# Weight remainders of the first nine chunks on TensorE and ScalarE, x(0) loaded in three parts, the second network's splits in block 1

## The reference

```python
w = np.exp(weight_gen - max); w = w / (w.sum(-1) + 1e-9)      # 8 heads x 7 taps
out[b,s,h] = sum_k w[b,s,h,k] * x_pad[b, s+k, h]              # x_pad: 6 zero rows ahead
xn = out / np.sqrt(np.mean(out * out, -1) + 1e-6) * rms_g
y = (silu(xn @ w_gate) * (xn @ w_val)) @ w_out                # 192 -> 1536 -> 192
h = y @ w_in                                                  # 192 -> 2048
z = (h * sigmoid(1.702 * h)) @ w_out2                         # 2048 -> 192
```

## Time and profile before

| | us |
|---|---|
| median of 3 runs (lowest, highest) | 1263.56 (1263.46, 1265.49) |
| profiled execution | 1263.64 |
| its span | 1261.9 |
| PE busy in the span | 1216.1 (96%) |
| DVE, ACT, POOL busy | 788.4, 680.8, 68.5 |

### The profile page before, as it was taken

The page is one execution under the profiler, slowest core; times in us unless marked ns, Lnnn a source line. Parts: engine busy times, 40 slices in busy tenths (PEclk is TensorE's granted clock), DMA queues, the critical chain, the costliest instruction groups (busy, mean ns, idle before and its releaser), DMA issues.

```text
span 1261.9 us, 28865 instructions
## 1 busy us (share of the span) xinstructions
PE 1216.1 (96%) x11968; PEld 1063.5 (84%) x11968; DVE 788.4 (62%) x1218; ACT 680.8 (54%) x1222; POOL 68.5 (5%) x67
## 2 busy tenths in 40 slices
PE   0889999999999999999999999999999999999998
PEld 0769999999888898988889888898988889888888
DVE  8868566484855749476474856648476574854532
ACT  3364655546465554656556455554656555464554
POOL 3760000000000000000000000000000000000000
PEclk9989999999999999999999999999999999999999
DMA  6230000010100001001010100001000000000000
GB/s 191 79 94 32 1 18 33 18 33 1 33 18 18 32 5 45 2 17 34 18 33 1 49 1 18 32 17 34 1 18 32 18 32 2 14 2 14 1 14 14
DMA packets 14625, 33.69 MB, mean 27 GB/s; under 512 B 1828, under 2 KB 7842, under 8 KB 14496
## 3 DMA queue, kind: packets, MB, share of 16 engines
q1 hardware_dynamic: 14496, 31.85, 7.8%
HBM read 25.55 MB, written 6.29 MB: 25 GB/s over the span
## 4 chain that ended last, share of the span: by engine, by line
PE 93%; DVE 4%; issue 1%; ACT 1%; POOL 1%; DMA 0%; SPq 0%; DVEq 0%; POOLq 0%; ACTq 0%
PE up_ps L808 49%; PE acc L808 37%; PE acc L812 4%; PE up_ps L812 3%; DVE mixed L627 1%; DVE tap L623 1%; DVE hidden L758 1%; DMA x_win<-in_x_dram 0%; DVE h_lo L767 0%; DVE normed_all L623 0%; POOL pair_lo L413 0%; PE acc L1051 0%; POOL out_w L413 0%; DVE mixed L623 0%; ACT up_w L446 0%
## 5 line engine op out<-in xcount | busy, mean ns | idle before, releaser
L767 DVE TENSOR_TENSOR h_lo<-hidden,h_hi 128x512 fp32r<-128x512 f32 x448 | 312.3, 697 | 359.2 <-ACT h_hi L545 357.7
L545 ACT CAST h_hi<-hidden 128x512 fp32r<-128x512 f32 x448 | 278.1, 621 | 250.1 <-DVE hidden L758 240.5
L808 PE MATMUL acc<-out_w,h_hi 64*128 64x384 f32 x1024 | 302.6, 355 | 1.0 <-DVE out_sb L714 1.0
L812 PE MATMUL acc<-out_w,h_hi 64*128 64x384 f32 x1024 | 302.4, 355 | 0.0
L538 ACT ACTIVATE hidden<-up_ps 128x512 f32<-128x512 f32 x256 | 152.7, 596 | 194.4 <-PE up_ps L812 194.3
L808 PE MATMUL acc<-out_w,h_lo 64*128 64x192 f32 x1024 | 255.0, 249 | 0.0
L812 PE MATMUL acc<-out_w,h_lo 64*128 64x192 f32 x1024 | 254.7, 249 | 0.0
L812 PE MATMUL up_ps<-x_hi,up_w 64*128 64x512 f32 x752 | 237.0, 394 | 0.0
L808 PE MATMUL up_ps<-x_hi,up_w 64*128 64x512 f32 x752 | 236.8, 394 | 0.0
L808 PE MATMUL acc<-h_hi,out_w 64*128 64x512 f32 x576 | 196.8, 394 | 9.1 <-POOL pair_lo L413 6.5
L812 PE MATMUL acc<-h_hi,out_w 64*128 64x512 f32 x576 | 197.4, 396 | 0.1
(11 more groups left out here) (111 smaller groups left out, 3219.2 us busy)
## 6 DMA issues: line engine op xcount, KB each, us to landing
x_win<-in_x_dram SPq DMA_DIRECT2D x14, 960.0 KB
out_dram<-out_sb SPq DMA_DIRECT2D x15, 384.0 KB, 2.3
stage<-in_moe_w_out_dram SPq DMA_DIRECT2D x13, 192.0 KB, 2.5
logits<-in_weight_gen_dram SPq DMA_DIRECT2D x16, 112.0 KB, 2.0
stage<-in_moe_w_in_dram SPq DMA_DIRECT2D x4, 256.0 KB, 2.6
stage<-in_moe_w_in_dram SPq DMA_DIRECT2D x8, 128.0 KB, 3.1
stage<-in_moe_w_gate_dram SPq DMA_DIRECT2D x3, 256.0 KB, 2.8
stage<-in_moe_w_gate_dram SPq DMA_DIRECT2D x6, 128.0 KB, 3.2
```

What stands on the lines that cost most here:

```text
L545: nc.scalar.copy(h_hi[:, u % 4, :], hidden[:, u % 2, :]).then_inc(hi_ready, 1)
L767: nc.vector.tensor_tensor(h_lo[:, u % 4, :], hidden[:, u % 2, :], h_hi[:, u % 4, :].bitcast(F32), ALU.subtract).then_inc(lo_ready, 1)
L808: return nc.tensor.matmul(ps, w[TOP], data[TOP], start=start, stop=stop)
L812: return nc.tensor.matmul(ps, w[LOW], data[LOW], start=start, stop=stop)
```

## The change

1. Chunks 0 to 8 (`BY_PE`): the remainder is no longer GpSimd's. TensorE multiplies the staged fp32 chunk by the identity into a bank of `up_ps` and adds the rounded chunk times the negated identity (`leave`), and ScalarE copies the bank to the `lo` tile (`chunk_lo`). On ScalarE rounding n alternates with remainder n - 1. GpSimd makes the negated identity and splits chunks 9 to 17 once x(0) is scaled.
2. x(0) comes in three parts (own rows; the three rows next to them; the three farthest), and its taps are mixed in reverse order, so that a tap waits for no more than it reads. A rest chunk is one transfer.
3. The mean is gone from VectorE: GpSimd adds the epsilon to the sum of squares ahead of its power, and g is scaled by the root of 192 once.
4. The main part of x(0) is turned and scaled before the rest part; its twin copy moves from VectorE to ScalarE. The first two taps of x(1) stand ahead of unit 0; the squares (6 to 5) and the turn of x(1) (10 to 9) move up by a unit.
5. The second network's chunks (18 to 33) are split in block 1, behind GpSimd's power for x(2). The last eight are loaded and rounded there too, behind the loads of x(2) and x(3) on SP; the first eight are rounded one to a unit in block 0.

```diff
     for k in range(2, TAPS):
         MIX += [f"mul{k}", f"add{k - 1}"]
-    MIX += [f"add{TAPS - 1}", "mean", "scale"]
+    MIX += [f"add{TAPS - 1}", "scale"]
...
-        return 48 * (g + 1) if g < 2 else g * 16 + 80
+        return 32 if g == 0 else g * 16 + 64
...
-                5: ["mul4", "add3"], 6: ["mul5", "add4"], 7: ["mul6", "add5"], 8: ["add6"], 9: ["mean"],
-                10: ["scale"]}
-    MIX_SLOT_0 = {0: ["mul0", "mul1"], 1: ["mul2", "add1"], 2: ["mul3", "add2"], 3: ["mul4", "add3"],
-                  4: ["mul5", "add4"], 5: ["mul6", "add5"], 6: ["add6"], 7: ["mean"], 8: ["scale"]}
-    EVAC_O, EVAC_Y0, SQUARE_0, SQUARE, SPLIT_Y, X_T = 1, 1, 6, 8, 8, U1 - 1
+                5: ["mul4", "add3"], 6: ["mul5", "add4"], 7: ["mul6", "add5"], 8: ["add6"], 10: ["scale"]}
+    AHEAD = ["mul0", "mul1"]
+    MIX_SLOT_0 = {0: ["mul2", "add1"], 1: ["mul3", "add2"], 2: ["mul4", "add3"], 3: ["mul5", "add4"],
+                  4: ["mul6", "add5"], 5: ["add6"], 7: ["scale"]}
+    EVAC_O, EVAC_Y0, SQUARE_0, SQUARE, SPLIT_Y, X_T = 1, 1, 5, 8, 8, U1 - 1
...
+    BY_PE = 9
+    HELD = CHUNKS1 + SLOTS
+    TURN_1 = U1 - 3
...
+    def hi_before(u):
+        if u < 0:
+            return SLOTS + LENT
+        return min(SLOTS + LENT + 2 * u + 2, CHUNKS1 + max(u - 2, 1), HELD)
...
+        def left_bank(n):
+            return up_ps[(n + 3) % 4]
...
+            def load_first_x():
+                sp.dma_start(x_win[:, HALO:, :], x_v[:, 0:STEP, :]).then_inc(own_in, 16)
+                for first, end, loaded in ((HALO // 2, HALO, near_in), (0, HALO // 2, x_in)):
+                    for b in range(B):
+                        lo, hi = b * BATCH_P, (b + 1) * BATCH_P - 1
+                        sp.dma_start(x_win[lo + 1:hi + 1, first:end, :],
+                                     x_v[lo:hi, OWN - HALO + first:OWN - HALO + end, :]).then_inc(loaded, 16)
...
-                    for half in range(2):
-                        sp.dma_start(to[half * REST:(half + 1) * REST, :],
-                                     w[P:D, c * COLS:(c + 1) * COLS]).then_inc(loaded, 16)
+                    twice = w[P:D, c * COLS:(c + 1) * COLS].unsqueeze(0).broadcast_to([2, REST, COLS])
+                    sp.dma_start(to, twice).then_inc(loaded, 16)
...
-            load_first_x(1)
+            load_second_x()
             load_logits(2)
-            for n in range(SLOTS + LENT, CHUNKS1 + SLOTS):
+            for n in range(SLOTS + LENT, HELD):
                 load_chunk(n)
             load_x(2)
-            for n in range(CHUNKS1 + SLOTS, len(chunks)):
-                load_chunk(n)
             load_logits(3)
             load_x(3)
+            for n in range(HELD, len(chunks)):
+                load_chunk(n)
             for i in range(2, GROUPS - 2):
...
+            pool.wait_ge(ident_ready, 1)
+            nc.gpsimd.tensor_scalar_mul(neg_ident[:, :], ident[:, :], -1.0).then_inc(neg_ready, 1)
+            pool.wait_ge(g_in, 48)
+            nc.gpsimd.tensor_scalar_mul(g_main[:, :], g_main[:, :], math.sqrt(D)).then_inc(g_ready, 1)
+            nc.gpsimd.tensor_scalar_mul(g_rest[:, :], g_rest[:, :], math.sqrt(D)).then_inc(g_ready, 1)
...
+            def rms(g):
+                pool.wait_ge(squared, g * STEP + STEP)
+                if g:
+                    pool.wait_ge(mix, mix_count(g - 1, "scale"))
+                nc.gpsimd.tensor_scalar_add(rms_stat[:, 1, :], rms_stat[:, 0, :], D * 1e-6).then_inc(summed, 1)
+                pool.wait_ge(summed, g + 1)
+                nc.gpsimd.tensor_tensor(rms_stat[:, 2, :], rms_stat[:, 1, :], neg_half[:, :],
+                                        ALU.pow).then_inc(rstd, 1)
+            rms(0)
+            pool.wait_ge(mix, mix_count(0, "scale"))
+            for n in range(BY_PE, CHUNKS1):
                 split_chunk(n)
-            pool.wait_ge(chunk_split, RMS0_AT)
-            rms(0)
-            pool.wait_ge(rstd, 1)
-            for n in range(RMS0_AT, RMS1_AT):
+            rms(1)
+            rms(2)
+            for n in range(CHUNKS1, len(chunks)):
                 split_chunk(n)
-            pool.wait_ge(chunk_split, RMS1_AT)
-            rms(1)
-            pool.wait_ge(rstd, 2)
-            for n in range(RMS1_AT, len(chunks)):
-                split_chunk(n)
-            pool.wait_ge(chunk_split, len(chunks))
-            for g in range(2, GROUPS):
+            for g in range(3, GROUPS):
                 rms(g)
...
+            def chunk_lo(n):
+                _, kind, t, _ = chunks[n]
+                act.wait_ge(chunk_left, n + 1)
+                for _, _, lo, f, _ in split_parts(left_bank(n)[:, :], kind, t):
+                    last = nc.scalar.copy(lo, f)
+                last.then_inc(chunk_split, 1)
...
+                else:
+                    act.wait_ge(rest_scaled, 1)
+                    nc.scalar.copy(y_twin[REST:P, :], x_f32[0:REST, 1, :]).then_inc(twin_ready, 1)
...
-                        for n in range(SLOTS + LENT + 2 * u, min(SLOTS + LENT + 2 * u + 2, len(chunks))):
+                        for n in range(hi_before(u - 1), hi_before(u)):
                             chunk_hi_half(n)
+                    if i == 1 and U1 <= u < U1 + len(chunks) - HELD:
+                        chunk_hi_half(HELD + u - U1)
...
-            for n in range(SLOTS + LENT - 4):
+            chunk_hi_half(0)
+            for n in range(1, BY_PE - 2):
                 chunk_hi_half(n)
+                chunk_lo(n - 1)
             mix_square(0)
             mix_exp(1)
-            for n in range(SLOTS + LENT - 4, SLOTS + LENT):
-                chunk_hi_half(n)
-            act.wait_ge(g_in, 48)
+            chunk_lo(BY_PE - 3)
+            chunk_hi_half(BY_PE - 2)
+            chunk_hi_half(BY_PE - 1)
+            act.wait_ge(g_ready, 2)
             scale_main(0)
             round_first(0)
+            chunk_lo(BY_PE - 2)
+            chunk_lo(BY_PE - 1)
+            for n in range(BY_PE, SLOTS + LENT):
+                chunk_hi_half(n)
...
+                        dve.wait_ge(soft, soft_count(g, "norm"))
+                    if g == 0 and k == 0:
+                        dve.wait_ge(own_in, 16)
+                    if g == 0 and k == 1:
+                        dve.wait_ge(near_in, 16 * B)
+                    if k == (HALO // 2 + 1 if g == 0 else 0):
                         dve.wait_ge(x_in, x_count(g))
-                        dve.wait_ge(soft, soft_count(g, "norm"))
                     if k == 3 and g:
...
-                    ins = nc.vector.tensor_tensor(*tap_product(to, k, 0, STEP), ALU.mult)
+                    ins = nc.vector.tensor_tensor(*tap_product(to, k if g else TAPS - 1 - k, 0, STEP), ALU.mult)
...
-            for step in MIX[:-2]:
+            for step in MIX[:-1]:
                 mix_step(0, step)
             mix_step(1, "max")
             mix_step(1, "sub")
-            mix_step(0, "mean")
             mix_step(0, "scale")
             for step in SOFT[2:]:
                 mix_step(1, step)
             split_first(0)
+            for step in AHEAD:
+                mix_step(1, step)
...
+                if i == 0 and p < 2 and k == 0:
+                    pe.wait_ge(chunk_split, BY_PE - 2 + p * 2)
...
+            def leave(n):
+                _, kind, t, _ = chunks[n]
+                src = places[place_of(n)]
+                if n >= 4:
+                    pe.wait_ge(chunk_split, n - 3)
+                if n == 0:
+                    pe.wait_ge(neg_ready, 1)
+                pe.wait_ge(chunk_hi, n + 1)
+                cols = 2 * D if kind == "out1" else COLS
+                nc.tensor.matmul(left_bank(n)[:, 0:cols], ident[:, :], src[:, 0:cols], start=True, stop=False)
+                parts = split_parts(left_bank(n)[:, :], kind, t)
+                for a, (_, to, _, _, _) in enumerate(parts):
+                    hi = parts[a][0]
+                    ins = nc.tensor.matmul(to, neg_ident[:, :], hi, start=False, stop=a == len(parts) - 1)
+                ins.then_inc(chunk_left, 1)
...
                     pe.wait_ge(ident_ready, 1)
-                elif g > 2:
+                    pe.wait_ge(main_normed, 1)
+                else:
+                    pe.wait_ge(mix, mix_count(g, "scale"))
...
+                if g == 0:
+                    ins.then_inc(main_turned, 1)
+                    pe.wait_ge(mix, mix_count(0, "scale"))
...
+            for n in range(BY_PE - 2):
+                leave(n)
             turn_x(0)
+            for n in range(BY_PE - 2, BY_PE):
+                leave(n)
```

52 lines of the change are left out of this document (25 added, 27 removed).

## The result

| | before | after |
|---|---|---|
| median of 10 runs (lowest, highest), us | 1264.68 (1262.77, 1265.77) | 1261.43 (1260.95, 1262.16) |
| profiled execution, its span, us | 1263.64, 1261.9 | 1260.95, 1259.2 |
| first product of block 0 | 39.08 | 42.18 |
| first product of block 1 | 95.47 | 88.99 |

The ratio is 0.9977 (95% interval 0.9967 to 0.9986): 3.3 us faster, a third of the 9.7 us forecast. The direction was right and the time, 1261.4, is at the very top of the range (1261.5), where it lies by luck: the range was drawn for cheap leaves and a cold start, and neither is what happened. The first unit came *later* than before, 42.18 us where 34.5 had been forecast.

The account below looks back on a forecast made before the run. TensorE was taken to bound the kernel from 100 us on, with the loss ahead of that, in start-up and block 0. Gains of 4.6 and 6.6 us less 1.5 in block 1 gave 9.7 us: 1254 us, range 1245 to 1261.5.

Parts of the forecast that it names:

- cheap leaves: Rival, start-up: fp32 matmul near its low bound, squares at 19.2 us, gain 14 to 20 us, about 1246 us; chance 0.17.
- cold start: Rival, start-up: array stays at 1.2 GHz or fp32 matmul takes 2.5 us; first product 39, time 1258.5 us; chance 0.16.
- the start-up: Up to block 0's first product: squares near 21.1 us, first product at 34.5 instead of 39.08, 4.6 us gained.
- The taps ahead of unit 0: Before block 0's first product: the first two taps of x(1) go ahead, hidden by TensorE's wait, at no cost.
- The leaves: Start-up, TensorE's work per remainder: fp32 matmul 1.7 us plus fp32r 0.42; 2.1 us a chunk cold, 1.1 warm.
- the price of 0.38: Block 0: each microsecond of GpSimd work costs VectorE 0.38 us; 13 us of splits cost 4.9, taken as 4.5.
- the row that was to show the product spared: Block 0: VectorE's product at 65.52 us, taking 0.68, cited as not blocked by GpSimd because one input is in PSUM.
- The unit of the turn: Near block 0's end, where x(1) is turned, after unit 9: 5.7 us instead of 7.8, product 10 at 75.0.
- the drain: From block 0's last product to block 1's first: 6.5 us (bounds 5 and 9) instead of 9.1, partly at full clock.
- Block 1: 22.3 us of GpSimd splits moved here; VectorE has 9.7 us free, 8.5 us fit unevenly; charged 1.5 us (0 to 5).
- block 1 pays: Rival, block 1: splits hold VectorE for their whole length, 13 us late plus 4 for the clock; 1269 us; chance 0.06.
- The rivals that ended near 1260: Remainders no earlier in start-up: 1258.5 us, chance 0.16. Late held chunks stall block 1 by 5 to 8: 1260 to 1263, 0.09.

Follow-up runs that it names:

- e1: The kernel after the change, with each rest chunk again loaded in two transfers of 64 rows: 1252.77 us, ratio to before 0.9914.
- e3: The kernel after the change, with each rest chunk one transfer of 128 different rows (wrong weights, only times of use): 1252.71 us.
- e4: e1 with the first two taps of x(1) back behind the products of unit 0, squares and scaling of x(1) one unit later: 1253.73 us.
- e9: e1 with GpSimd's subtractions for the second network's chunks cut to one element a row, waits and order kept: 1249.12 us.
- e6: e1 with all the second network's splits in block 1 held until after VectorE's scaling of x(2): 1252.3 us.

## Why the prediction was right or wrong

**The step that failed** is one sentence of the start-up: "The chunk transfers still wait for all of x(0), so chunk 0 still reaches ScalarE at about 11.1 and chunk 6 at about 17.7 us". It carried the chunks' old times over to transfers of another form. The description of the change names the single transfer, but the prediction gave it no cost and no bound, so no rival held it. Measured, chunk 0 was there at 10.36, but chunk 1 at 16.36 and chunk 3 at 22.26, the squares started at 28.23 instead of 21.1, the first product at 42.18 instead of 34.5. e1 takes just this away: squares 21.69, first product 33.03, and 1252.8 us against the 1254 of the sum. That the time is so near is in part luck: in e1 the first product is 1.5 us sooner than forecast and block 0 is 3.0 us shorter, while block 1 loses 2.4 us more than charged (all below). e3 and the DMA share narrow the cause to the shape of the broadcast transfer.

**The taps ahead of unit 0** were "hidden by TensorE's wait". They were not in the change, since x(1) came last in the queue that the rest chunks held up: silu of unit 0 ran from 39.69 to 40.29, and the taps held the product to 42.18. The term was right on the condition that x(1) is there (e4: a gain of 1.0 us). The prediction named no such condition. This is the same failed step seen a second time.

**The leaves** (a chunk times the identity plus the rounded chunk times the negated one) came out near their sum, by luck. Leaves 1 and 2 of the kernel after start 2.30 us apart at the slow pace, against 2.1 forecast. But the fp32 product takes 1.09 us of it (17.03 to 18.12), not 1.7, and the fp32r product 1.21 (18.12 to 19.33), not the 0.42 of a product on 64 rows; here it is on all 128:

```profile
17.03 2.08 PE L1108 MATMUL up_ps<-stage,ident 128*128 128x512 f32 x2 [3.44 <-ACT up_w L472]
18.12 1.42 PE L1112 MATMUL up_ps<-up_w,neg_ident 128*128 128x512 f32 x1
19.33 1.91 PE L1108 MATMUL up_ps<-stage,ident 128*128 128x512 f32 x2
```

At the fast pace a leaf takes 1.19 us (leaves 7 and 8 of e1, 26.08 to 28.46), against 1.1 forecast. Leaves 7 and 8 were counted at the slow pace, 4.2 us. The change bears that out (32.61 to 36.66, 4.05 us, granted clock 0.50 from 34 to 36 us); e1, with its 2.38 us at a clock of 1.00, doesn't, and this makes its first product 1.5 us sooner than 34.5.

The squares of e1, 0.6 us past the forecast, bear out the chain of seven roundings and six remainders. The scaling without a split beside it took 0.69 + 0.42, where 1.3 had been estimated.

**Block 0.** From the first product to block 1's first was forecast at 49.8 us and took 46.8, in the change and in e1 (33.03 to 79.86) alike. The five mixing units came out at 20.3 us (42.18 to 62.52; 20.9 forecast). That does not prove the price of 0.38: the last of them, with GpSimd idle from 59.98, took 2.94 us (59.58 to 62.52) and not 3.28, so against that pace GpSimd's 12.52 us in this stretch cost 5.6 us, 0.45 us per microsecond. Nor does the row that was to show the product spared do so: GpSimd is idle at 65.52 in before. The product at 61.54 does, 0.67 us beside a split that runs from 60.88 to 62.50. The four after them took 11.3 us instead of 13.9: units 6 to 8 follow each other in 2.3 to 2.4 us (66.17, 68.46, 70.85), where 3.28 had been put for every unit. TensorE itself is busy all of these 11.33 us and begins its units 3.3 us apart, so the products catch up on banks that it had filled while VectorE was late:

```profile
63.07 0.40 PE L860 MATMUL up_ps<-y_hi,up_w 64*128 64x512 f32 x1
...
66.35 0.40 PE L860 MATMUL up_ps<-y_hi,up_w 64*128 64x512 f32 x1
```

The sum had no such term. The unit of the turn took 5.26 us (5.7 forecast), the one after it 2.71 (2.8) and the drain 7.2 (6.5). The drain's mechanism was the one forecast, a higher clock than before; here are the drains of before and of the change:

```profile
86.39:95.47 9.08, 6.92 (x38) 5.96 (x40) 1.38 (x2) 4.58 (x6) 3.76 (x4) 0.65 0.01 2
```

```profile
81.82:88.99 7.17, 6.95 (x47) 5.66 (x48) 1.37 (x4) 4.17 (x5) 0.00 (x0) 1.00 0.06 16
```

TensorE also waits less for GpSimd's remainders, in before and then in the change (total us, times, longest):

```profile
PE acc L808 <- POOL pair_lo L413: 6.5, 3, 4.0
...
PE up_ps L808 <- POOL out_w L413: 1.6, 1, 1.6
```

```profile
PE acc L860 <- POOL pair_lo L435: 2.0, 1, 2.0
```

**Block 1** was charged 1.5 us within 0 to 5; it is 3.9 us longer in the change than in before (78.81 and 74.88 us), and e9 puts 3.1 to 3.6 of it down to the splits. The mechanism is the one given, GpSimd's work stretching VectorE's in the gated units 9 to 11. The size failed because 0.38 us per GpSimd microsecond, an average over five units, was set against 9.7 us of free time in a 25 us window. The splits instead fall on the split of y (122.11, 1.50) and the scaling (124.94, 1.48) where VectorE has no slack. The rival *block 1 pays* had this mechanism and the wrong size (13 us and more). The second network's waits for GpSimd, put at nothing, were indeed covered in the change (the one wait for GpSimd left is in block 0, at 50.03); they come up only when the splits are moved back (e6, 2.2 us).

**The sum again.** Start-up 7.7 us late, block 0 3.0 us less: block 1's first product at 88.99 instead of 84.3, 4.7 us. Block 1: 2.4 us more than charged. Together 7.1, against the 7.0 us between the span's 2.7 us of gain and the 9.7 forecast. The rivals that ended near 1260 gave other reasons for it: that the remainders are slow (no, e1), or that held chunks come late (no wait of TensorE for them in block 1). Their times were near the measured one, their causes were not there.
